# Clips moved to the end of the slot in front, fewer bridging products and a later division in the start-up of a three-part kernel

## The reference

```python
# q, k, v: (2, 8, 576, 64): batch, heads, sequence, head size
scores = scale * np.matmul(q, k.transpose(0, 1, 3, 2))
kth = np.partition(scores, -32, axis=-1)[..., -32:-31]
scores = np.where(scores >= kth, scores, -1e9)
attn = softmax(scores);  attn_out = attn @ v
# tokens x 512, then a gated layer: 512 -> 1536 -> 512
xn = x / sqrt(mean(x * x) + 1e-6) * rms_g
x = (silu(xn @ w_gate) * (xn @ w_val)) @ w_out
# then 8 experts, each token to the one with the largest logit,
# 512 -> 1024 -> 512, scaled by its softmax probability, up to 288 rows an expert
```

## Time and profile before

| what | us |
|---|---|
| median of three runs | 640.18 |
| lowest and highest of them | 639.88 and 641.45 |
| the profiled execution's own time | 640.57 |
| its span, first to last instruction | 638.8 |
| PE busy in it | 611.8 |
| DVE busy in it | 411.5 |
| ACT busy in it | 328.6 |
| POOL busy in it | 265.3 |

### The profile page before, as it was taken

How to read it: one execution, slowest core, us unless ns; L and a number is a source line. 1 busy time by engine, 2 the same in 40 slices (tenths; PEclk the granted TensorE clock), 3 DMA queues, 4 the chain that set the end, 5 groups by cost and what they waited for, 6 DMA issues and landing times.

```text
span 638.8 us, 11148 instructions
## 1 busy us (share of the span) xinstructions
PE 611.8 (96%) x3935; PEld 470.0 (74%) x3935; DVE 411.5 (64%) x912; ACT 328.6 (51%) x713; POOL 265.3 (42%) x375
## 2 busy tenths in 40 slices
PE   7799989999999999999999999999999999999994
PEld 5466765875766766766766757757589999999994
DVE  5999999899898997998998998902011111011110
ACT  4777877766767766767756757653110110111100
POOL 1866875464365464553654555542310110011101
PEclk9899999999999999999999999999999999999998
DMA  9999800000000000000000000000696776766501
GB/s 239 214 360 337 244 14 0 16 20 2 17 18 1 18 18 2 16 18 2 18 18 2 1 18 2 9 9 1 211 384 185 263 270 208 279 216 235 174 2 39
DMA packets 55182, 65.45 MB, mean 102 GB/s; under 512 B 32282, under 2 KB 32282, under 8 KB 55132
## 3 DMA queue, kind: packets, MB, share of 16 engines
q1 hardware_dynamic: 53388, 60.05, 29.5%
q0 software_dynamic: 1744, 4.76, 2.0%
HBM read 52.89 MB, written 12.30 MB: 102 GB/s over the span
## 4 chain that ended last, share of the span: by engine, by line
PE 91%; ACT 3%; POOL 2%; issue 1%; DMA 1%; SPq 1%; DVE 0%; POOLq 0%; ACTq 0%
PE ps L574 14%; PE ps L869 12%; PE ps L855 11%; PE ps L526 7%; PE ps L533 7%; PE ps L527 7%; PE ps L507 7%; PE ps L480 6%; PE ps L491 6%; PE ps L465 4%; PE ps L589 2%; DMA w_loads<-in_moe_w_gate 1%; PE ps L702 1%; PE ps L880 1%; ACT pt L928 1%
## 5 line engine op out<-in xcount | busy, mean ns | idle before, releaser
L1563 POOL TENSOR_TENSOR s_ring<-s_ring,z_pair 128x576 f32<-128x576 f32 x72 | 100.7, 1420 | 68.9 <-ACT z_pair L1063 68.9
L1374 DVE MATCH_REPLACE8 w_top<-m,w_top 128x576 f32<-128x576 f32 x144 | 105.7, 741 | 0.0
L1368 DVE MAX8 m<-w_top 128x8 f32<-128x576 f32 x144 | 101.5, 745 | 0.0
L574 PE MATMUL ps<-wo_space,hid 128*128 128x512 f32 x216 | 100.7, 593 | 0.8 <-issue 0.8
L526 PE MATMUL ps<-w_parts,x_hi 128*128 128x512 f32 x196 | 81.7, 417 | 0.0
L527 PE MATMUL ps<-w_parts,x_hi 128*128 128x512 f32 x196 | 77.5, 395 | 0.0
L869 PE MATMUL ps<-arena,w_loads 128*128 128x168 f32 x512 | 75.8, 307 | 0.6 <-issue 0.6
L1588 POOL DMA_INDIRECT out_rows<-arena,s_ring x16 | 15.1, 941 | 147.0 <-DVE arena L1398 144.5
L855 PE MATMUL ps<-arena,w_loads 128*128 128x168 f32 x512 | 74.3, 306 | 0.6 <-ACT arena L928 0.6
L855 PEld LDWEIGHTS ps<-arena,w_loads 128*128 128x128 f32 x512 | 73.3, 190 | 0.9 <-ACT arena L928 0.9
L869 PEld LDWEIGHTS ps<-arena,w_loads 128*128 128x128 f32 x512 | 73.2, 190 | 0.8 <-issue 0.8
(11 more groups left out here) (143 smaller groups left out, 877.8 us busy)
## 6 DMA issues: line engine op xcount, KB each, us to landing
w_loads<-in_moe_w SPq DMA_DIRECT2D x16, 2048.0 KB, 8.9
dispatched_rows<-drow SPq DMA_DIRECT2D x18, 260.0 KB, 7.1
w_loads<-in_moe_w_gate SPq DMA_DIRECT2D x3, 1024.0 KB, 7.7
w_loads<-in_moe_w_val SPq DMA_DIRECT2D x3, 1024.0 KB, 9.9
wo_space<-in_moe_w_out SPq DMA_DIRECT2D x1, 3072.0 KB, 11.5
arena<-dispatched_rows SPq DMA_DIRECT2D x8, 341.2 KB
out_rows<-drow SPq DMA_DIRECT2D x9, 256.0 KB, 5.2
q_space<-in_q SPq DMA_DIRECT2D x8, 256.0 KB, 3.3
```

What stands on the lines that cost most here:

```text
L574: last = mm(blk[0], hid[:, c * P:(c + 1) * P], wo_s[:, c, :], start=(c == 0), stop=(c == CF - 1))
L1368: vec.max(m8[:, 2 * (n % 2) + a, i, :], w_top[:, a, :]).then_inc(s["top_step"], 1)
L1374: vec.match_replace(w_top[:, a, :], m8[:, 2 * (n % 2) + a, i, :], w_top[:, a, :], NEG).then_inc(s["top_step"], 1)
L1563: gp.tensor_tensor(row, row, z_pair[:, a, :], ALU.subtract).then_inc(s["lowered"], 1)
```

## The change

It changes three things, all in slots 0 to 4.

1. Bridging products: behind the scores 10, 1, 2 and 3 of them in slots 1, 2, 3 and 4, instead of 10, 3, 3 and 3; behind the values 1, 2 and 2 in slots 1, 2 and 3, instead of 2 each.
2. ACT's clips of pairs 1, 2 and 3 move from slots 2, 3 and 4, where they stood behind the output columns, to the end of slots 1, 2 and 3. In slot 1 they stand behind the weight pieces of GAMMA, in slots 2 and 3 ahead of them. The clips of pair 0 stay in slot 1.
3. On POOL the division of slot 3 moves behind the weight piece that is due there.

```diff
--- before.py
+++ after.py
@@ -38,7 +38,7 @@
 ALPHA, BETA, GAMMA, MARKS = 0, 1, 2, 3
 
 START = (4, 2, 1)
-EARLY = (10, 3)
+EARLY = (10, 1, 2, 3)
 AWAKE = (1, 2)
 
 XA, XB = -4, -3
@@ -773,7 +773,7 @@
                         pe.wait_ge(s["k_acted"], KC - 1)
                         if g > 1:
                             pe.wait_ge(s["k1_copied"], min(2 * g - 2, KC))
-                        bridge(EARLY[g > 0])
+                        bridge(EARLY[g])
                     early = n - FIRST + 1 if n in (FIRST, FIRST + 1) else None
                     if early:
                         first_block((wg_hi, wg_lo), early, blk[1])
@@ -823,7 +823,7 @@
                     if g < HP - 1:
                         if g > 0:
                             pe.wait_ge(s["k1_copied"], min(2 * g, KC))
-                        bridge(2)
+                        bridge(2 if g > 0 else 1)
                 turn_first_rows(n)
 
             first_rows(2)
@@ -1138,9 +1138,10 @@
                 elif n <= HP:
                     if g > 0:
                         out_columns(g - 1)
-                    if here:
+                    if g == 0:
                         marks(g, 0)
                         marks(g, 1)
+                    if here:
                         probs(g, 0)
                     score_rows(n + 1, 0)
                     if here:
@@ -1163,7 +1164,13 @@
 
                             act.wait_ge(s["k_turned"], KC + i + 1)
                             keys(1, i, blk[i % 2]).then_inc(s["k1_copied"], 1)
-                    dense(n, GAMMA)
+                    if n == 1:
+                        dense(n, GAMMA)
+                    if 0 < n < HP:
+                        marks(n, 0)
+                        marks(n, 1)
+                    if n != 1:
+                        dense(n, GAMMA)
                 else:
                     if 0 <= g - 1 < NG:
                         out_columns(g - 1)
@@ -1565,9 +1572,9 @@
                     norm_last(t)
                 if t is not None:
                     rms(t)
+                dense(n, ALPHA)
                 if n == HP - 1:
                     divide(0, 0, 0, H - 2)
-                dense(n, ALPHA)
                 dense(n, BETA)
                 dense(n, GAMMA)
                 t = due(n, GAMMA, XA)
```

## The result

The changed kernel took 641.30 us (median of 20 runs, 640.55 to 644.04), the kernel before 639.94 us beside it (20 runs, 639.34 to 641.47). The ratio is 1.0020, with a 95% interval of 1.0011 to 1.0028: slower by 1.3 us, which is clear of no change, and inside the 0.3% that the prediction called the same. The 20 times of the changed kernel fall into two groups: 13 from 640.55 to 641.40 and 7 from 642.05 up. The profiled execution took 642.05 us, with a span of 640.2 us, so the profile shows one of the second, smaller group.

What follows compares the result with a forecast made beforehand. VectorE's search and TensorE's matrix work were taken to share the bound, with 0.66 us of DVE idle time to win. Parts summed 0 + 0.1 + 0 = +0.1 us on the median 640.18, forecasting 640.3 us, range 639.4 to 641.6.

Steps and rivals of the forecast that it cites:

- the sum: Over the three parts of the change: 0 + 0.1 + 0 = +0.1 us, part 2 ranging from 0 to 0.28.
- DVE's gap before the second maximum of pair 5: DVE's only printed idle time before 60 us, 0.66 us before 59.33; the most the change could take off DVE.
- Part 2: Clips moved to the slot in front: scores of pair 5 start at 51.51, at most 51.77, against 51.49; +0.1 us.
- So it is there at about 48.15: End of slot 3: ACT reaches the clips of pair 3 at about 48.15, 0.6 us to spare before they can start.
- rival D: ACT's copies make it late at the clips of pair 3; gap stays 0.66, 640.2 us; chance 0.05.
- Rival B: New PE idle time makes TensorE's clock fall between 47 and 51 us, adding 2.7 us: 642.9; chance 0.06.
- Rival C: First low clock stretch lies elsewhere or lasts longer in unprofiled runs; changed kernel loses 0.7 to 1.9 us less; chance 0.05.
- Part 1: Four fewer bridging products in slots 1 to 3, none removed in slot 4: 0 us on the path making the gap.
- part 3: POOL's division behind weight part 6 in slot 3: ends at about 46.7, frees POOL at 48.46; 0 us.
- Rival A: DVE's gap closes, 0.66 us, 639.5, if the scores of pair 5 start at 50.85 or earlier; chance 0.12.

Runs made afterwards that it cites:

- e11: Changed kernel with the clips of pairs 1 and 2 back in their old places, only those of pair 3 moved; 642.96 us, ratio to before 1.0029.
- e12: Changed kernel with the clips of pair 3 back at the start of slot 4; 640.24 us, ratio to before 1.0006.
- b2: Kernel before, run once more with no edit for a second profile; 639.98 us, ratio 1.0002.
- e10: Changed kernel with five bridging products instead of two behind the values of pair 1, covering PE's wait; 640.95 us, ratio to before 1.0018.
- e1: Kernel before with only the fewer bridging products, clips and division in their old places; 639.92 us, ratio to before 1.0001.
- e4: Changed kernel with ACT copying the output columns ahead of the clips in slots 2 and 3; 639.77 us, ratio to before 1.0000.
- e5: Changed kernel with output columns ahead of the clips in slots 2 and 3 and the old bridging products; 640.14 us, ratio to before 1.0001.
- e6: Changed kernel with weight parts 6 and 7 ahead of the clips of pairs 2 and 3; 640.24 us, ratio to before 1.0000.
- a2: Changed kernel, run once more with no edit for a second profile; 641.20 us, ratio to before 1.0022.

## Why the prediction was right, and where its working was off

The range and the class "the same" were right: 641.30 lies in 639.4 to 641.6 and within 0.3%. The time itself was 1.0 us over the forecast of 640.3, and the change over before was +1.36 us (medians; +1.3 by the ratio) where the sum had +0.1 and at most +0.28. That the range held it is partly luck: its upper end came not from the mechanism, whose sum ended at 640.5, but from 1.3 us allowed for an unlucky median of few runs. The sum's miss of 1.0 us used up most of that allowance.

- **The bound and its size.** That DVE's gap before the second maximum of pair 5 is the place of action, and that it is made by a chain which begins with the scores of pair 5, is shown by the nine profiles that have a gap: in seven of them the gap is the start of these scores, counted from the first search, less 41.1 us, and in e11 the fall of the clock lengthens the chain behind them, in e12 VectorE was already 0.2 us late. That 0.66 us was the most to win was read from one execution, and it was off twice. In that execution DVE lost time in two more places behind the gap, and its start-up was 1.23 us longer than in b2. And in its second profile the kernel before has no gap at all, so there was nothing to win in a typical execution: the three kernels whose scores of pair 5 start before 40.5 take the same time as before.
- **Part 2, the term of the sum.** The working of the wait itself was exact: threshold, clips, part 7, output columns and PE's start were summed to 51.51, that is 41.80 after the first search and 2.79 after the start of the clips; the kernel with the covered wait shows 41.87 and 2.79. What failed is the subtraction: "at most 51.77, against 51.49 before" should have been against 40.57 + 9.71 = 50.28. That makes the term +1.23 us in place of +0.1, and it measured +1.0 (640.95 against 639.94; ratio 1.0018, 1.0008 to 1.0028). The old place of the clips had let the output columns through first, which left PE more room than one profile showed. A slip without effect: the scores wait for the output columns of three pairs earlier, not two.
- **"So it is there at about 48.15".** This step failed outright. ACT reached the clips of pair 3 at 50.18, since slot 3 was late and not early. I had priced the idle time of PE before the scores of pair 4 at 1.1 us; it was 2.59 and 2.40 us in the two profiles. These scores themselves came where the sum had them (32.26 us after the first search, forecast 41.85 - 9.71 = 32.14): PE was there earlier than reckoned, and the clock fell. Without the fall, in e10, ACT did stand waiting at the clips of pair 3. Clips later than 49.5 were also the sign named for rival D; but no transfer of keys made them so (PE transposed them at its lower clock, at 46.82, without waiting), and the time was not D's 640.2.
- **Rival B** was the right mechanism in the wrong slot and too large: the clock did fall, in slot 3 and for 3.4 us, in both profiles. In the profiled executions it made the start-up 0.9 to 1.0 us longer, and the medians differ by 0.25 to 0.35 us, which is not clear of noise; the rival had 2.7. The argument against it left out most of the idle time above. Its price was also mis-summed: 6.8 us of low clock from 47 ends at 53.8 and leaves 2.3 us behind 51.5, half of which is 1.15 and not 1.6; from 50.6 it is 2.95 and not 2.7. Only with the clips of pair 3 alone did the fall reach the chain of slot 4, and there it cost 1.64 us of PE's time.
- **Rival C** had the first low stretch of another length, and this was so: 3.4 to 10.2 us. Its gain did not come, since before does not wait there in a typical execution.
- **Part 1** (the fewer products cost nothing) and **part 3** (nor does the division) were right, by the two kernels that have them alone. The clock stood the fewer products as long as PE did not also have to wait. The Trainium skill (TensorE: Matmul & The Clock Gate, Part 4: PE-mode transpose) says that transposes don't count as busy time of PE in the same way. In the kernel with the fewer products alone 8.3 of PE's 23.05 busy us from 30.76 to 57.20 are transposes, and the granted clock there is 1.00. The products that stay are in it too, so this does not refute the page.
- **Rival A** needed the weight part out of the way, it said. With the weight parts ahead, the loss is gone by the median (640.24, ratio 1.0000), but nothing is won over before, since a typical execution has no gap to close.

No version beat both kernels: the lowest median, 639.77 with the output columns first, can't be told from before (1.0000, 0.9991 to 1.0008). The start-up is 100.3 us in it as in the second profile of before: DVE searches without a break in both.

## What to carry to other kernels

An instruction moved ahead in an engine's queue takes its wait along, and everything behind it waits too: here clips that needed a threshold held up a copy of 0.3 us that was ready, and that copy was what the next engine stood still for. Put what is ready and awaited ahead of what has to wait. And before a stall of a few tenths is taken as the gain to be had, look at a second execution: one profile may hold a stall that the typical run lacks.

## What the runs showed of the hardware

- The first low stretch of TensorE's clock lasted 3.4, 6.8 or 10.2 us in the fourteen profiles, and 6.8 or 3.4 us for one and the same changed kernel.
- A second low stretch came in all four profiles in which PE had been wholly idle for 2.40 to 3.04 us at once, beginning between 0.4 us before and 1.5 us after the end of that idle time, and in none of those in which its longest idle time in slots 2 to 4 was 0.74 to 1.33 us. That is no limit below which idle time is safe: the first low stretch came in all fourteen, and in thirteen of them no idle time of the 10 us in front of it was over 1.41 us, but several followed one another (1.38, 1.28 and 0.84 us in e1; 2.12 us was the longest in the first profile of before).
- What such an idle time cost depended on where the low stretch fell: 0.9 to 1.0 us of the start-up in slot 3 with a fall of 3.4 us, 1.64 us in slot 4.
- The start of the first search was at 9.71 to 11.54 us, and most of this seems to be PE's own speed. The transposes of the queries, which wait for a transfer, began at 6.34 to 6.79 us in all fourteen profiles. But the four records at L465 took 0.62 to 0.70 us in four of them (first search at 9.71 to 10.19) and 1.06 to 1.12 in the others, and the eight records of the first scores took 1.98, 2.29 and 2.21 us in e4, e5 and e6, against 1.24 to 1.29 in the eleven others. These three are the ones with the first search at 11.36 to 11.54. At the granted clock of 0.50 eight such records took 2.29 us (42.56 in a2), at 1.00 1.24 us (42.38 in the changed kernel). So I take it that PE was at its lower level for longer there; this rests on the durations alone, since the view by stretches gives a granted clock of 1.00 even from 2.00 to 12.10 in e5. The spread of 1.8 us is as large as that of most times of one kernel.
